# Three chained blocks on one core: values for the block means turned, x turned in chunks, row-wise maxima, nine weight places, shorter routing, first item in parts

## The chip, the cores and the metric

One core of one Trainium2 chip runs the whole program in one launch. The metric is device microseconds (us) of that core from start to end; lower is better. The engines are TensorE (PE, with its weight loads as PEld), VectorE (DVE), ScalarE (ACT), GpSimd (POOL) and SyncE (SP), which here only issues transfers. All of them run their own instruction streams and meet at semaphores.

## The reference

Three blocks follow each other; each takes what the one before gives. The sizes are B=4, H=8, S=768, D=64 for attention, N=3072 tokens of 512 for the two expert blocks, 8 experts of 512x1024 and 1024x512, and 32 slots.

```python
# attention: a local band and 24 block summaries
k_sum = k.reshape(B, H, nb, 32, D).max(axis=3)
v_sum = v.reshape(B, H, nb, 32, D).mean(axis=3)
scores_l = scale * q @ k^T, kept where |i - j| < 16
scores_s = scale * q @ k_sum^T + log(32)
a = softmax over both together;  x = a @ [v, v_sum]
# soft mixture: slots are softmax-weighted means of tokens, per column
logits = x @ phi
d = softmax over tokens (axis 0);  slot_input = d.T @ x
slot_out[e] = relu(slot_input[e] @ w1[e]) @ w2[e]
x = softmax over slots (axis 1) @ slot_out
# switch: one expert per token, gated by its probability
logits = normalised x @ normalised expert_emb.T / tau
out[mask_e] = gate * (relu(x[mask_e] @ w1b[e]) @ w2b[e])
```

## The kernel before

**Attention.** Per batch the 8 heads go as 4 pairs, each pair as 3 steps (NSTEP = 12 a batch, 48 in all). A step scores 4 tiles of 128 rows against 96 near keys and 24 block keys (120 columns). On PE a step is: scores of step s+2 (a mask product and 8 small ones, L539, L547), the transposes of the probabilities of s+1 (L556), the products with the values of s (L569). DVE takes the row maximum (L949), scales it (L953) and, when the products are there, divides (L970 to L977). ACT does the exponentials (L806) and the copy of the transposed probabilities (L814). So each step passes PE, DVE, ACT, PE, ACT, PE, and scores run two steps ahead. The block maxima of keys are taken by DVE (L944) and spread by POOL into gaps between the key windows (L455, "gaps_filled").

**Block sums of v.** They come from a second copy of v laid out by block (v_by_block, 96 partitions of 16384 B a batch). DVE halves one part for the first batch; POOL halves the rest (L439) and spreads the sums (L449). Then SP copies them into rows 48 to 72 of every value window by DMA (load_sums, L341); for this the windows are loaded in two pieces of 48 partitions (L327, L328).

**The order of transfers.** All of them are issued by SP in one program order. A wait on one holds up all behind it. Keys and queries of pair p of batch b (L320) wait until the scores of the same pair one batch earlier are done, values until its products are done. The weights are 16 units of 2 MB in a ring of 8 places (load_unit, L262); units 0 to 3 are issued inside attention, 4 when the scores of the last pair but one are over, 5 to 7 once the logits are done, 8 to 15 as soft_up and the second product free places.

**Soft mixture.** PE turns x (96 transposes, L598), waits for all copies, and multiplies with phi (L605). The maximum of each slot over all tokens is a maximum per row, turned, reduced and sent back (L612 to L618) before the exponentials (L834). They are turned (L621), copied, multiplied with x (L630). Then per pair of experts: soft_up (L659), relu, transposes, second product (L700). The exponentials of the combine weights, their transposes and a copy (L843) stand before the first soft_up.

**Switch routing.** A Gram matrix and logits of slots (L716), then products with the combine weights (L723) give the squared norm and the logits of each token; the norms, the softmax and the choice of expert are made in one row of DVE instructions (L1081 to L1100), then counted (L727), then the list of experts used is made (L1109 to L1126, experts_ready), and only then SP loads w1b of that expert (L389) and, behind it, w2b.

**Items.** An item is 256 tokens of one expert. In these inputs all tokens go to one expert, so n_used is 1 and there are 12 items. The inner matrices are folded, g = slot_out @ w1b (L744), and split into a high and a low part for three products in the fast 32-bit form (L774, 24 for each tile of 128 tokens); hidden is L760. w2b is split the same way by ACT (L910) and DVE (L1202). Items are walked by each_item: a loop over 8 groups of 12 with a branch for each group and each item. Each finished tile is gated by ACT (L876) and scattered by POOL (L516).

## Time and profile before

| | |
|---|---|
| median of 3 runs | 481.75 us (481.75 to 485.83) |
| the profiled execution | 482.98 us, its span 481.2 us |
| granted clock, mean over the span | 0.865 |
| PE busy | 347.4 us, 72% |
| DVE, ACT, POOL busy | 191.3, 147.2, 73.9 us |
| HBM read | 68.91 MB |
| chain that ended last | PE 52%, DMA 25%, DVE 9% |

The rows further down are of four kinds. A stage table has, for each stretch of the span, the busy time of each engine with its number of instructions, the granted clock of TensorE (1 is 2.4 GHz, 0.5 is 1.2 GHz), the busy share of the DMA engines and what they moved. The chain of waits is the one line of work, followed back from the end, that set the end; a DMA row in it is time in which everything waited for that transfer. A timeline lists the instructions of one engine with their start and length, and in brackets how long the engine was idle before and who ended it.

### The profile page before, as it was taken

The page shows a single profiled execution, that of the slowest core. Times are in us where ns is not written, and L with a number is a line of the kernel's source. Part 1 is how long each engine was busy: PE and PEld are TensorE (multiplying, and loading weights), DVE is VectorE, ACT ScalarE, POOL GpSimd, SP SyncE. Part 2 cuts the span into 40 slices and gives each one's busy share as a digit, 9 for nine tenths or more (in the row PEclk, how much of TensorE's full clock was granted, in tenths as well). Part 3 has the DMA queues.
Part 4 walks back from the last instruction along what each step waited for, and adds up shares of the span by engine and source line. Part 5 has one row for each costly group of instructions (what it writes and reads, how often), then busy time and mean ns, then how long its engine had stood idle before and what let it go on. Part 6 is the DMA issues. An engine that isn't in the chain of part 4 may idle for free.

```text
span 481.2 us, 8929 instructions
## 1 busy us (share of the span) xinstructions
PE 347.4 (72%) x3119; PEld 243.7 (51%) x3120; DVE 191.3 (40%) x435; ACT 147.2 (31%) x329; POOL 73.9 (15%) x103
## 2 busy tenths in 40 slices
PE   0516737399689697958871850438999999999991
PEld 0314525266456465733320330117888888888880
DVE  1614435268777477443110138263222222222221
ACT  1203325066367375341200011052222222222221
POOL 3302600811710030000000000000111111111110
PEclk9967768599799799977977895567999999999997
DMA  8999999979999822076799800900111111111110
GB/s 228 254 250 290 386 227 216 224 199 240 229 243 315 196 94 84 1 268 256 293 377 406 320 1 0 330 22 1 44 44 44 44 44 44 44 44 47 49 49 29
DMA packets 23174, 77.90 MB, mean 162 GB/s; under 512 B 2376, under 2 KB 3528, under 8 KB 22768
## 3 DMA queue, kind: packets, MB, share of 16 engines
q1 hardware_dynamic: 21232, 71.31, 50.5%
q0 software_dynamic: 1920, 6.29, 3.4%
q8 instruction: 14, 0.23, 0.2%
q14 instruction: 8, 0.07, 0.0%
HBM read 68.91 MB, written 6.29 MB: 156 GB/s over the span
## 4 chain that ended last, share of the span: by engine, by line
PE 52%; DMA 25%; DVE 9%; issue 4%; ACT 3%; SPq 3%; POOL 1%; DVEq 0%; ACTq 0%; POOLq 0%
PE ps L774 28%; DMA ring<-ring 9%; DMA ring<-in_qk 8%; DMA ring<-in_moe_w 6%; DMA ring<-vsum 3%; PE ps L569 3%; PE ps L659 3%; PE ps L760 2%; PE ps L556 2%; PE ps L700 2%; PE ps L547 2%; DVE small L949 2%; PE ps L598 2%; ACT work L806 2%; PE ps L630 2%
## 5 line engine op out<-in xcount | busy, mean ns | idle before, releaser
L806 ACT ACTIVATE work<-ps,small 128x120 f32<-128x120 f32 x192 | 53.4, 361 | 106.2 <-DVE small L953 106.1
L774 PE MATMUL ps<-high_w2b,hid_high 128*128 x192 | 76.0, 396 | 4.7 <-DVE hid_low L1176 4.7
L774 PE MATMUL ps<-low_w2b,hid_high 128*128 x192 | 75.7, 394 | 0.0
L774 PE MATMUL ps<-high_w2b,hid_low 128*128 x192 | 75.4, 393 | 0.0
L1176 DVE SCALAR_TENSOR_TENSOR hid_low<-ps,hid_high 128x1024 fp32r<-128x1024 f32 x26 | 31.8, 1225 | 61.8 <-ACT hid_high L894 61.8
L569 PE MATMUL ps<-ring,work 120*64 120x65 f32 x768 | 37.4, 247 | 25.6 <-DMA ring<-ring 15.3
L556 PE MATMUL ps<-ident,work 128*120 128x128 f32 x192 | 35.4, 313 | 19.7 <-ACT work L806 19.2
L516 POOL DMA_INDIRECT out_x<-work,small x24 | 23.5, 979 | 166.9 <-DVE small L1169 59.6
L876 ACT ACTIVATE work<-ps,small 128x512 f32<-128x512 f32 x24 | 16.5, 688 | 104.3 <-PE ps L774 104.3
L569 PEld LDWEIGHTS ps<-ring,work 120*64 120x64 f32 x768 | 30.3, 155 | 35.1 <-issue 27.0
L774 PEld LDWEIGHTS ps<-high_w2b,hid_high 128*128 128x128 f32 x192 | 36.6, 191 | 12.2 <-issue 5.0
L774 PEld LDWEIGHTS ps<-high_w2b,hid_low 128*128 128x128 f32 x192 | 36.6, 190 | 7.9
L774 PEld LDWEIGHTS ps<-low_w2b,hid_high 128*128 128x128 f32 x192 | 36.7, 191 | 7.2
L556 PEld LDWEIGHTS ps<-ident,work 128*120 128x120 f32 x192 | 22.5, 152 | 30.7 <-ACT work L806 26.6
L949 DVE TENSOR_REDUCE small<-ps 128x4 f32<-128x480 f32 x48 | 31.4, 655 | 13.8 <-PE ps L547 13.2
L539 PE MATMUL ps<-work,ident_bf 128*128 128x240 bf16 x96 | 21.0, 307 | 21.8 <-POOL ring L455 21.8
L547 PE MATMUL ps<-ring 64*64 64x120 f32 x768 | 36.5, 314 | 0.0
L439 POOL TENSOR_TENSOR ring<-ring 96x512 f32<-96x512 f32 (+5 forms) x16 | 29.5, 1842 | 34.9 <-DMA ring<-in_v_by_block 34.2
L659 PE MATMUL ps<-ring,small 128*32 128x512 f32 x128 | 20.7, 812 | 15.0 <-DMA ring<-in_moe_w 14.4
L547 PEld LDWEIGHTS ps<-ring 64*64 64x64 f32 x768 | 23.7, 155 | 12.1 <-issue 12.1
L814 ACT ACTIVATE work<-ps 120x512 f32<-120x512 f32 x48 | 29.5, 614 | 0.3 <-PE ps L556 0.3
L1165 DVE CAST g_stage<-g_parts 128x1024 fp32r x14 | 9.7, 694 | 47.8 <-PE ps L760 46.0
(193 smaller groups left out, 339.8 us busy)
## 6 DMA issues: line engine op xcount, KB each, us to landing
ring<-in_moe_w SPq DMA_DIRECT2D x17, 2048.0 KB, 14.9
ring<-in_qk SPq DMA_DIRECT2D x16, 928.0 KB, 16.7
ring<-in_v SPq DMA_DIRECT2D x32, 292.5 KB
ring<-in_v_by_block SPq DMA_DIRECT2D x4, 1536.0 KB, 14.1
whole_w2b<-in_moe_w SPq DMA_DIRECT2D x1, 2048.0 KB, 12.6
ring<-ring SPq DMA_DIRECT2D x12, 146.2 KB
ring<-vsum SPq DMA_DIRECT2D x4, 146.2 KB
out_x<-work,small POOLq DMA_INDIRECT x24, 2.7
```

The costliest lines, as they stand in the source:

```text
L439: link(pool.tensor_tensor(left, left, right, ALU.add))
L516: pool.indirect_dma_start(out, bass.IndirectOffsetOnAxis(id_buf[u], 0), o_sb[u], None, bounds_check=NTOK - 1, oob_is_err=False).then_inc(r ...
L539: pe.matmul(sc[u][:, h, 0:2 * KC], ident_bf[:, :], mask[:, 2 * g:2 * g + 2, :].rearrange("p i c -> p (i c)"), start=True, stop=False, skip ...
L547: last = pe.matmul(sc[u][par * QT:(par + 1) * QT, h, ii * KC:(ii + 1) * KC], qT[pair][rows, (2 * i + par) * QT:(2 * i + par + 1) * QT], kT ...
L556: last = pe.transpose(pt[s % 2][0:KC, j, :], probs[s % 2][:, j, :], ident[:, :])
L569: last = pe.matmul(av_of(u, h, ii)[par * QT:(par + 1) * QT, :], probsT[u][0:KC, 2 * h + ii, par * QT:(par + 1) * QT], v_win[pair][0:KC, t, ...
L659: last = pe.matmul(ps[j * SLOTS:(j + 1) * SLOTS, pr % 2, :], siT[:, c, :], as_w1(4 * pr + j // 2)[:, c, (j % 2) * BANK:(j % 2 + 1) * BANK] ...
L774: last = pe.matmul(ps[:, 4 + u, :], hidden_part[:, u, m * P:(m + 1) * P], matrix[:, bass.ds(e * UNIT + m * DM, DM)], start=m == 0 and i == ...
L806: last = act.activation(probs[u][:, j, :], sc[u][:, j // 2, (j % 2) * KC:(j % 2 + 1) * KC], ACT.Exp, bias=negmax[u][:, j:j + 1], scale=flo ...
L814: act.activation(probsT[s % 2][0:KC, :, :], pt[s % 2][0:KC, :, :], ACT.Copy).then_inc(pT_ready, 1)
L949: dve.tensor_reduce(topscore[s % 2].rearrange("p (h i) -> p h i", h=2), sc[s % 2][:, :, 0:2 * KC].rearrange("p h (i c) -> p h i c", i=2), ...
L1176: dve.scalar_tensor_tensor(hid_low[:, u, :].rearrange("p (m t) -> p m t", t=P), hidden_of(u), 0.0, hid_high[:, u, :].rearrange("p (m t) -> ...
```

## The change

- **v turned.** The copy of v by block is replaced by one with the head dimension on 128 partitions (vt, 3072 B a row). DVE halves the first pair, POOL the other 15 (halve). PE turns the 24 sums of a pair (sums_by_block), DVE copies them (copy_block_sums), POOL writes them into the windows (fill_sums). No sums go by DMA.
- **Windows.** Value windows are loaded as one piece of 128 partitions. The stride of the key windows is 120 in place of 88, so a row of queries and keys is 8832 B in place of 7424 B; the block keys stand behind each window.
- **Masks and maxima.** The mask product is 4 quarter-array products in place of 2 full ones. The unscaled maximum lies in PSUM. The 1e-9 comes from a 121st row, so one DVE instruction goes from each step.
- **Issue.** ACT issues the first two vt loads, emb, tau and phi. Units 0 and 1 go after pair 1 and pair 2 of batch 1, 2 and 3 behind the last attention load; there is a ninth place for unit 8, in the space of x.
- **x in chunks.** The transposes of one chunk of 128 columns are followed by the logits of an earlier chunk; the first two stand inside the last two attention steps.
- **Row-wise maxima.** Exponentials use the maximum of their own row and read PSUM; a factor per row sets them to the common maximum later. The combine weights are made behind the first second product.
- **Routing.** The expert is chosen from logits without norms; the first expert is known from one short reduction, and its w1b is loaded in 4 parts, w2b in 4 more. Norms and gates come after the split of w2b.
- **First item.** Its first tile does all high-high products, then low-high, then high-low. keep_at_work adds products whose result nobody reads (5, 4, 2 and 1 of them).
- **Loops.** each_rank and each_item branch once for the case of one expert.

```diff
-            def load_blocks(b):
-                if b > 1:
-                    sp.wait_ge(vsum_pool, b)
-                sp.dma_start(v_blk, v_by_block[b].rearrange("p (j d) -> p j d", j=BLOCK)).then_inc(vblk_loaded, 16)
...
-                rows = v[b, pair].rearrange("p (t d) -> p t d", t=NT)
-                sp.dma_start(v_win[pair][0:FIRST, :, :], rows[0:FIRST]).then_inc(v_loaded[pair], 16)
-                sp.dma_start(v_win[pair][FIRST + NB:KC, :, :], rows[FIRST:WK]).then_inc(v_loaded[pair], 16)
...
-                sp.dma_start(v_win[pair][FIRST:FIRST + NB, :, :], source).then_inc(v_loaded[pair], 16)
+                sp.dma_start(v_win[pair], v[b, pair].rearrange("p (t d) -> p t d", t=NT))\
+                    .then_inc(v_loaded[pair], 16)
...
+                if n >= 2:
+                    if n > 2:
+                        sp.wait_ge(vb_ready, n - 2)
+                    else:
+                        sp.wait_ge(first_vb, 1)
+                    sp.dma_start(vT[n % 2], vt[b, pair]).then_inc(vT_loaded[n % 2], 16)
...
+            def halve(n):
+                pool.wait_ge(vT_loaded[n % 2], n // 2 * 16 + 16)
+                if n >= 2:
+                    pool.wait_ge(vsum_done, n - 1)
+                t = vT[n % 2]
+                for w in (16 * NB, 8 * NB, 4 * NB, 2 * NB):
+                    link(pool.tensor_tensor(t[:, 0:w], t[:, 0:w], t[:, w:2 * w], ALU.add))
+                pool.tensor_tensor(vb[n % 2][:, 0:NB], t[:, 0:NB], t[:, NB:2 * NB], ALU.add).then_inc(vb_ready, 1)
...
-        topscore = [small[:, 1032 + 4 * u:1036 + 4 * u] for u in range(2)]
+        topscore = [flat[:, (2 * u + 1) * BANK - 4:(2 * u + 1) * BANK] for u in range(2)]
...
+            def keep_at_work(bank, times):
+                for _ in range(times):
+                    pe.matmul(ps[:, bank, :], ident[:, :], comb[:, 0:BANK // SLOTS, :].rearrange("p q s -> p (q s)"),
+                              start=True, stop=True)
...
-            with eng.Fori(0, E) as c:
-                with eng.If(c * NPT < n_items):
-                    with eng.Fori(0, NPT) as j:
-                        with eng.If(c * NPT + j < n_items):
-                            body(c * NPT + j)
+            with eng.Fori(1 if head else 0, NPT) as j:
+                body(j)
+            with eng.If(n_items > NPT):
...
+                elif kidx == 7:
+                    sp.wait_ge(logits_part, DC)
+                elif kidx == RING:
+                    sp.wait_ge(si_done, 1)
+                else:
+                    p = kidx - RING - 1
+                    if p % 4 < 2:
+                        sp.wait_ge(h_done, p // 4 + 1)
+                    else:
+                        sp.wait_ge(so_done, p // 4 + 1)
...
-            act.activation(E_sb, L_sb, ACT.Exp, bias=nmax, accum_out=zpart).then_inc(e_ready, 1)
+            act.activation(E_sb, flat[:, 4 * BANK:4 * BANK + S], ACT.Exp, bias=nmax, accum_out=zpart).then_inc(e_ready, 1)
...
+                for i, (hidden_part, matrix) in enumerate(((high, high_m), (low, high_m), (high, low_m))):
```

The queue of SP before, in batch 1 from behind pair 1 to behind pair 2 ("in_v" are the two pieces of the value window, the ring<-ring row is the copy of the sums):

```order
L315 DMA ring<-in_v_by_block 96x4096 [waits vsum_pool]
L320 DMA ring<-in_qk 128x1856 [waits scores_done]
L327 DMA ring<-in_v 48x1560 [waits av_done]
L328 DMA ring<-in_v 48x1560
L341 DMA ring<-ring 24x1560 [waits vsum_spread,av_done] x3
```

and the start of batch 1 now (in_vt is the turned v; its two places are in the ring and in comb):

```order
L341 DMA ring<-in_qk 128x2208 [waits scores_done]
L351 DMA ring<-in_vt 128x768 [waits vb_ready]
L357 DMA ring<-in_v 128x1560 [waits av_done]
L341 DMA ring<-in_qk 128x2208 [waits scores_done]
L351 DMA comb<-in_vt 128x768 [waits vb_ready]
L357 DMA ring<-in_v 128x1560 [waits av_done]
L277 DMA ring<-in_moe_w 128x4x1024
```

A pair has three transfers of 128 partitions in place of one of 128, two of 48 and one of 24, with one of 96 for each batch; and a vt load waits for POOL's halving two pairs earlier.

PE at the end of attention before (L569 are products with the values, L598 transposes of x, L605 logits):

```order
L556 MATMUL ps<-ident,work 120x128 x4
L569 MATMUL ps<-ring,work 64x65 x16
L598 MATMUL ps<-ident,x_or_g 128x128 x96
L605 MATMUL ps<-ring,phi_sb 32x512 x4
L605 MATMUL ps<-ring,phi_sb 32x256 x4
```

and now (L611 are the products with the values, L624 the transposes, L632 the logits):

```order
L581 MATMUL ps<-ident,work 120x128 x4
L624 MATMUL ps<-ident,x_or_g 128x128 x6
L611 MATMUL ps<-ring,work 64x65 x8
L624 MATMUL ps<-ident,x_or_g 128x128 x6
L611 MATMUL ps<-ring,work 64x65 x8
L624 MATMUL ps<-ident,x_or_g 128x128 x36
L632 MATMUL ps<-work,phi_sb 32x512 x4
L632 MATMUL ps<-work,phi_sb 32x256 x4
L624 MATMUL ps<-ident,x_or_g 128x128 x24
```

Twelve transposes moved ahead of the last products with values, and the other 84 are mixed with the logits.

DVE from the logits of the tokens to the first expert now (before, 35 DVE instructions stand from the same point, L1081, to experts_ready at L1126):

```order
L1248 TENSOR_REDUCE small<-ps 128x24 [waits y_done]
L1249 TENSOR_TENSOR small<-ps,small 128x192 [waits dve_seq]
L1256 TENSOR_REDUCE small<-ps 1x8 [waits count_done,codes_ready]
L1257 SCALAR_TENSOR_TENSOR work<-small 1x8 [waits dve_seq]
L1258 TENSOR_REDUCE small<-work 1x1 [waits dve_seq]
L1259 TENSOR_SCALAR en_home<-small 1x1 [waits dve_seq]
```

Six instructions now stand between them; the norms and gates have moved behind the split of w2b.

## Rows read from the trace of the kernel before

**Rows 1.** Stage table: stretch, busy us (instructions) by engine, clock, DMA share, GB/s.

```profile
34.00:186.00 152.00, 112.19 (x1758) 78.15 (x1760) 89.68 (x243) 73.01 (x227) 41.53 (x53) 0.83 0.90 236
186.00:206.00 20.00, 16.82 (x172) 12.99 (x166) 11.34 (x22) 7.33 (x10) 0.00 (x0) 1.00 0.00 1
206.00:225.00 19.00, 12.68 (x88) 6.35 (x91) 7.98 (x16) 6.24 (x9) 0.00 (x0) 0.82 0.91 331
225.00:281.00 56.00, 40.22 (x296) 13.51 (x295) 6.58 (x12) 4.32 (x7) 0.00 (x0) 0.82 0.80 301
281.00:301.00 20.00, 4.48 (x54) 3.50 (x54) 13.86 (x48) 3.75 (x5) 0.41 (x2) 0.72 0.00 1
301.00:338.00 37.00, 21.49 (x76) 13.76 (x77) 14.09 (x22) 8.84 (x10) 1.09 (x1) 0.64 0.32 115
```

**Rows 2.** Chain of waits in attention: start, length, what.

```profile
21.98 15.04 DMA ring<-vsum
39.01 27.39 DMA ring<-in_qk
73.41 18.73 DMA ring<-ring
```

**Rows 3.** Stage table, single stretches while attention loads or weights are in flight.

```profile
13.00:14.00 1.00, 0.00 (x0) 0.00 (x0) 0.65 (x1) 0.00 (x0) 0.00 (x0) 1.00 1.03 198
16.00:17.00 1.00, 1.00 (x17) 0.70 (x16) 1.00 (x1) 0.00 (x0) 0.96 (x1) 1.00 1.02 423
28.00:29.00 1.00, 0.00 (x0) 0.00 (x0) 0.00 (x0) 0.00 (x0) 0.00 (x0) 0.50 0.99 402
45.00:60.00 15.00, 9.28 (x134) 6.28 (x135) 5.85 (x13) 4.92 (x16) 11.46 (x8) 0.77 1.05 392
```

**Rows 4.** Timeline of PE, first products with values.

```profile
34.04 1.13 PE L569 MATMUL ps<-ring,work 120*64 120x65 f32 x16 [10.29 <-DMA ring<-vsum]
```

**Rows 5.** Timeline of ACT: exponentials of steps, two stretches without a transfer wait.

```profile
99.63 1.11 ACT L806 ACTIVATE work<-ps,small 128x120 f32<-128x120 f32 x4 [2.03 <-DVE small L953]
...
115.66 1.11 ACT L806 ACTIVATE work<-ps,small 128x120 f32<-128x120 f32 x4 [1.04 <-DVE small L953]
...
176.76 1.11 ACT L806 ACTIVATE work<-ps,small 128x120 f32<-128x120 f32 x4 [0.77 <-DVE small L953]
...
183.12 1.11 ACT L806 ACTIVATE work<-ps,small 128x120 f32<-128x120 f32 x4 [0.48 <-DVE small L953]
```

**Rows 6.** Timelines of POOL and DVE at the same moment.

```profile
119.51 4.51 POOL L439 TENSOR_TENSOR ring<-ring 96x2048 f32<-96x2048 f32 x1 [2.53 <-DMA ring<-in_v_by_block]
...
119.73 4.32 DVE L953 TENSOR_SCALAR small<-small 128x4 f32<-128x4 f32 x1
```

**Rows 7.** Groups by line and form: busy, mean ns, idle before.

```profile
L439 POOL TENSOR_TENSOR ring<-ring 96x512 f32<-96x512 f32 x4 | 5.3, 1334 | 0.2
L449 POOL COPY ring<-vsum 96x1560 f32<-96x1560 f32 x3 | 4.4, 1480 | 9.0 <-DMA ring<-ring 8.9
L953 DVE TENSOR_SCALAR small<-small 128x4 f32<-128x4 f32 x48 | 16.6, 346 | 1.7
```

**Rows 8.** Timeline of PE: transposes of x.

```profile
191.42 8.08 PE L598 MATMUL ps<-ident,x_or_g 128*128 128x128 f32 x72 [0.89 <-DVE ring L1018]
```

**Rows 9.** Chain of waits, last two pairs of experts.

```profile
246.30 18.96 DMA ring<-in_moe_w
265.39 5.56 PE ps L659 x32
```

**Rows 10.** Timelines of SP, PE and DVE from the load of w1b on.

```profile
300.73 0.39 SPq L389 DMA_DIRECT2D ring<-in_moe_w  x1
308.62 6.15 PE L744 MATMUL ps<-ring,soT 128*64 128x512 f32 x16 [5.12 <-DMA ring<-in_moe_w]
319.21 4.62 DVE L1202 TENSOR_TENSOR low_w2b<-whole_w2b,high_w2b 128x1024 fp32r<-128x1024 f32 x4
```

**Rows 11.** Chain of waits, one item of 12.

```profile
346.85 10.91 PE ps L774 x48
```

More of the change, by code:

```diff
@@ L110, in attention_soft_moe_switch_moe @@
         x_sb = x_or_g[:, :].rearrange("p (b t d) -> p b t d", b=B, t=TT)
+        vb = [small[:, 1416 + SLAB * u:1416 + SLAB * (u + 1)] for u in range(2)]
         L_sb = work[:, 0:768]
@@ L704, in _ @@
                 last.then_inc(so_done, 1)
+                if pr == 0:
+                    comb_T()
+                for n in range(NCT):
+                    if ct_turn(n) == pr:
+                        if n == 1:
+                            embeddings_T()
+                        combine_T(n)
+                if 1 <= pr < E // 2 - 1:
+                    soft_up(pr + 1)
             pe.wait_ge(so_ready, 1)
@@ L724, in _ @@
             last.then_inc(y_done, 1)
[L726 to L727 removed]
+            pe.wait_ge(topped, 1)
+            pe.matmul(ps[:, 6, 0:NI], ones_bf[:, :], onehot.rearrange("p q e -> p (q e)"),
                       start=True, stop=True).then_inc(count_done, 1)
[L730 to L733 removed]
@@ new lines, in _, with list_T @@
+            for t in range(TT):
+                last = pe.matmul(flat[:, 4 * BANK + t * P:4 * BANK + (t + 1) * P], combT[:, t * P:(t + 1) * P],
+                                 gram_bd.rearrange("p b s -> p (b s)"), start=True, stop=True)
+            last.then_inc(gram_done, 1)
+            keep_at_work(3, 4)
+            def list_T():
+                pe.wait_ge(items_ready, 1)
+                for kind in range(3):
+                    last = pe.matmul(ps[0:1, 6, kind * P:(kind + 1) * P], item[:, kind:kind + 1],
+                                     ident[:, :], start=True, stop=True)
+                last.then_inc(list_done, 1)
@@ new lines, in _ @@
+            with dve.If(n_used < FEW + 1):
+                low_of_w2b(0, 0)
+                stage(1, (g_low_ready, n_used * 2))
+                low_part(0, 0)
+                for c in range(1, 4):
+                    low_of_w2b(0, c)
+                low_part(0, 1)
+                with dve.If(n_used > 1):
+                    for r in range(1, FEW):
+                        with dve.If(n_used > r):
+                            for c in range(4):
+                                low_of_w2b(r, c)
@@ L1208, in _ @@
+            with dve.If(n_used < FEW + 1):
                 each_item(dve, one_item(low_part))
             with dve.If(n_used > FEW):
-                stage(1, (hid_done, 1))
-                for u in range(2):
-                    second_half(0, u)
                 each_item(dve, one_item(second_half))
```

887 lines of the change are left out of this document (498 added, 389 removed).

## Prediction

> **What bounds the kernel now.** I read the stage table first, to cut the span where the limits change [rows 1]. Attention runs to 186, with the DMA engines 90% busy at only 236 GB/s while PE is busy 112 of 152 us. Turning x and the logits take until 206, soft routing until 225, the expert weights until 281 (80% DMA share at 301 GB/s), the choice of expert until the load of w1b at 300.7 [rows 10], the first item until 338. Then the items fill PE, 48 products in 10.91 us [rows 11] and the hidden ones between them, 143 us in all; the change leaves these products alone.
>
> Next the chain of waits in attention [rows 2]: one wait of 15.0 us for sums going by DMA, one of 27.4 us for keys, and one of 18.7 us for copies of sums, the longest of three (one for each later batch). So transfers set the end there, not arithmetic. Where no transfer is waited for, steps start 2.29 us apart (7 steps in 16.03) or 2.12 us (3 steps in 6.36) [rows 5].
>
> Why only 236 GB/s: the single stretches [rows 3] alternate. Keys and queries, 128 partitions high, come at 423 and 402 GB/s and the weights at 392, but in between, when by issue order the value pieces of 48 partitions are moving, it is 198. The Trainium skill, "SBUF — State Buffer", section "Door 1: The DMA port swizzle", says that partitions 0 to 63 lie on 8 of the 16 ports and 64 to 127 on the others, so that a piece of 48 gets about half the rate; the trace agrees (198 against 423). The same page puts HBM at about 358 GB/s for a core, and here the measurement, 392 over 15 us, decides; by the page attention would end some 6 us later than below.
>
> **The change part by part.** Against the span of 481.2 us.
>
> *Transfers of attention.* A pair loads keys and queries 8832 B x 128 = 1.13 MB, values 6240 B x 128 = 0.80 MB, vt 3072 B x 128 = 0.39 MB: 2.32 MB, in all 37.2 MB, against 33.5 MB now (0.95 + 0.60 + 0.15 a pair and 1.57 a batch). More bytes, but all in transfers of 128 partitions. At the 402 of rows 3 a pair takes 5.8 us, less than its three steps. With units 0 and 1 (2.1 MB each) it is 41.4 MB, 103 us, over by about 106, while the last pair is wanted near 119. So the waits of rows 2 go, and the loop of steps is what bounds next.
>
> *The loop of steps.* Per pair DVE loses three instructions on the sums and gains one copy of sums; PE gains one turning product; the quarter-array mask products cost between nothing and what they now cost. These go together; I take 2.25 us a step, near the 2.29 which has the block maximum in it. Bounds 2.12 and 2.45.
>
> *Start.* PE stood ready for the first products at 34.04 - 10.29 = 23.75 [rows 4]. Ahead of and with the first keys 2.5 MB had to land at about 200 GB/s, 12.6 us; now 1.9 MB at 402, 4.8 us. That gives 16, and the first sums add some 2 us: 18. Bounds 16 and 21. The last products end at 18 + 47 x 2.25 + 0.7 = 124.5. Gain 61.5.
>
> *POOL.* It is moved into every pair: 744 elements of additions at 2.6 ns (1334 ns for 512 [rows 7]) are 1.9 us, the copy of sums 1.5 us, the gaps 0.4: about 4 us of 6.75, so it does not bound. Behind each halving SP holds a vt load and all loads after it, but two pairs (13 us) lie between them.
>
> *x and logits.* 84 transposes instead of 96 remain (8.08/72 = 0.112 us each [rows 8], -1.3 us), and PE is idle 3.2 of these 20 us [rows 1], waiting for DVE at the start, for banks and for all copies before the logits; 2.7 of it goes. Gain 4, bounds 2 and 5.
>
> *Soft routing.* 19 us [rows 1]. A copy, a table load and half of another copy leave the path; at ACT's mean there (6.24/9 = 0.7, the table load about twice that) this is 2.5. DVE's round trip for the common maximum goes from it (two instructions at 7.98/16 = 0.5), and six transposes of combine weights trade places with six of logits. This sums to 3.5; PE stands idle for less time before the products with x and is at the low clock for less of them (mean 0.82 now), so 4.5. Bounds 2 and 6.
>
> *Expert weights.* Unit 8 starts at the end of the products with x. From the first soft_up (T) it is 3.8 us to its end, then units 9 to 15, 7 x 2.1 MB at 402 = 36.6 us, about 2 us to land: T + 42.4. Before, the chain waited 18.96 us for unit 13 and ran 15.6 us on PE behind it to 281 [rows 9]. Now unit 13 lands at T + 32, its soft_up takes 5.56 us cold or 3.6 warm, turning and copies 2.3, then five unread products of 0.85 (twice that at the low clock), ending T + 44; then 3.6 us: T + 48 against T + 56. Gain 8. The unread products cost about 2 us here, since the last weights land earlier; without this cover, up to 6. Bounds 4 and 11.
>
> *Choice of expert and first item.* DVE's 35 instructions between logits and list become 6 before the first expert is known. From 281 to the load of w1b at 300.7 it was 19.7 us, of which DVE 13.86 in 48 instructions, 0.29 each [rows 1]. Now some 9 of them are on the path (2.6), with 3.8 of products and 1.1 for SP: 7.5. The parts land until 7.8 us after the issue, so of the 6.15 us of products behind it [rows 10] only the last quarter is left, under 1.5 us. Then hidden, its high part, and four low parts of w2b (4.62 us [rows 10]) bound the first tile, done 20 us after the issue; the second needs its low part at 21 and ends at 27.5. **A wait is added:** behind that low part DVE has about 18 small instructions for ids, norms and gates (near 7 us), and everything of item 1 is queued behind them, so item 1 starts at about 32, with PE idle for 4 to 5 us. Before it was 37.3. Both together gain 12.2 + 5.3 = 17.5; I take 15.5 for a low clock after that idle time. Bounds 9 and 20.
>
> *End.* The seven branches of empty item groups behind the last item go; no row prices a branch, so I bound it by nothing and 4 us (the last product ends about 10 us before the span does) and take 2.
>
> Sum: 61.5 + 4 + 4.5 + 8 + 15.5 + 2 = 95.5. The span goes to 385.7; with 1.8 us around it the profiled execution would be 387.5. It lies 1.2 us above the median of 481.75, so 386 for the median.
>
> **The rivals.**
>
> *The value rows are slow in themselves.* 6240 B is no multiple of 256, and 198 GB/s was never seen on another length with 128 partitions. Then a pair takes 2.8 + 4.0 + 1.0 = 7.8 us, with two units 135 us, attention ends at 149 and the total is 411. For it: the new windows have the same row length; against it: the halves explain the number. 0.10.
>
> *POOL holds DVE.* A scaling of 128x4 maxima took 4.32 us beside a POOL addition of 4.51 [rows 6]; its mean is 346 ns [rows 7]. With POOL busy in 60% of each step at instructions of up to 1.5 us, a hold of 0.3 us on average at each of 48 steps, on the loop's path, makes 15 us: 401. The change puts the maxima into PSUM. The Trainium skill, "SBUF — State Buffer", section "Who interferes with whom", says that a VectorE instruction with at most one SBUF input outside the two-port modes does not contend with GpSimd; by that rule this rival falls, but no run here shows it for this operand. 0.11.
>
> *Slower than before: the low clock through the items.* The stretch of the first item is at 0.64 [rows 1], and I expect a new idle time before item 1. If TensorE stayed at 1.2 GHz, each item would take another 10.9 us, 131 in all: 517. It decides when over 96/131, 73% of the items, run so. Against it: the 48 products go at 0.227 us each [rows 11] without a gap, and nothing in the loop of items changed. 0.02.
>
> *The gains do not chain* (loads late in a place I have not seen, the unread products worse): 0.05, spread over 395 to 440.
>
> **How the numbers follow.** The forecast has 0.72 and gives 386. Its own range from the bounds, not all at one end, is 370 to 402. The low end stays; the high end takes in the first two rivals: 370 to 411. A measurement of this kernel can tell about 1% from no change, so same is 477 to 487. Faster 0.96, same 0.01, slower 0.03.
>
> **What would show it.** In the profile after: no wait for sums or keys in the chain of attention, step starts 2.1 to 2.4 us apart throughout, the last products near 125; the short stretches near 400 GB/s whenever loads run; DVE's scaling well under its mean of 346 ns beside POOL; the last weights landing before the fifth unread product ends; PE idle 4 to 5 us before item 1. It would be wrong if value loads stay near 200 GB/s, or if steps take over 2.5 us with no transfer in the chain.

## The result, and the profile after

The kernel after takes 386.12 us (median of 4 runs, 383.76 to 389.18), the kernel before 482.88 (481.75 to 485.83): ratio 0.799, 95% interval 0.792 to 0.807. Forecast were 386.0 and a span of 385.7; the profiled execution spans 385.7. The sum came out closer than its terms did. Some executions of any kernel run in a slower state, and ratios here and below compare the fast ones alone. The kernel before was run again beside each series of experiments, with medians from 482.9 to 485.7 us, and the kernel after was not. So a microsecond or two between kernels of different series is not to be read as their edits'; where it matters, the lines of the profiles are compared instead.

The stage table of after stands beside [rows 1]; its columns are the same, cut where the same stages now end.

```profile
0.00:16.00 16.00, 6.80 (x74) 4.38 (x75) 6.37 (x15) 4.92 (x15) 9.76 (x29) 1.00 0.84 319
16.00:123.00 107.00, 95.95 (x1895) 72.09 (x1894) 79.14 (x214) 73.70 (x229) 67.20 (x126) 0.98 1.02 412
123.00:139.00 16.00, 15.19 (x148) 10.71 (x147) 9.53 (x13) 5.68 (x7) 0.00 (x0) 1.00 0.49 183
139.00:151.00 12.00, 9.30 (x81) 4.45 (x81) 3.57 (x12) 3.04 (x7) 0.00 (x0) 1.00 0.66 210
151.00:201.20 50.20, 42.81 (x316) 14.91 (x308) 13.26 (x27) 7.74 (x12) 0.00 (x0) 0.93 0.87 327
201.20:209.00 7.80, 5.54 (x65) 5.20 (x65) 3.45 (x16) 0.60 (x1) 0.42 (x2) 0.80 0.00 0
209.00:245.70 36.70, 28.07 (x104) 15.87 (x103) 23.17 (x55) 11.43 (x15) 1.13 (x1) 0.90 0.32 116
245.70:385.70 140.00, 132.35 (x616) 110.67 (x616) 37.17 (x56) 37.12 (x45) 22.37 (x24) 0.98 0.12 45
```

Second line: attention is now 107 us, the transfers run at 412 GB/s without a break, and PE is busy 96 of them. The low mean of 236 GB/s is gone, and so are the long waits of [rows 2]. The chain of waits of after (start, length, what) has two transfers left in attention, one at the start and one of vt:

```profile
1.38 9.30 DMA comb<-in_vt
...
16.02 1.07 PE ps L611 x16
...
35.44 12.61 DMA ring<-in_vt
48.17 1.01 POOL ring L484
```

First value products at 16.02, against a forecast of 18 (34.04 before, [rows 4]); the last start at 122.29, 47 steps later, 2.26 us each. The second transfer is where the pace broke once: TensorE stood still 1.6 us near 50 and then ran at the low clock until about 56 (granted clock 0.56 from 53 to 56). Behind the hitch, from 63.63 to 122.22, 27 steps go at 2.17 us each.

From the second pair of soft experts on, the same chain reads:

```profile
169.20 6.55 PE ps L764 x32
...
191.64 0.67 PE ps L754 x4
...
193.07 4.56 PE ps L704 x10
197.63 3.62 PE ps L764 x32
...
208.86 0.36 SPq L401
...
210.88 6.81 DMA ring<-in_moe_w
...
217.74 0.81 PE ps L812 x6
218.55 1.01 PE ps L827 x4
219.56 3.75 issue
223.31 3.44 PE ps L704 x4
226.75 0.96 PE ps L857 x8
...
239.01 0.37 DVE small L1388
...
243.98 1.23 DVE hid_low L1331
...
245.68 4.57 PE ps L871 x12
```

Between the first soft_up at 150.73 and the choice of expert the chain has no transfer at all: TensorE and VectorE set the pace there, and the second product at 169.20 runs at the low clock, 6.55 us instead of the 3.64 of the others. `193.07 4.56 PE ps L704 x10` are the five unread products, whole on the chain; the prediction counted them and put 2 us on them. `219.56 3.75 issue` answers to nothing in the prediction. It is time in which TensorE waited for nothing that the profile shows, and behind it unread products at half speed (3.44 us instead of 1.98) push the first hidden tile from about 222 to 226. The last lines are the wait that the prediction named: item 1 starts at 245.68, after 4.19 us of idle TensorE (timeline of PE):

```profile
245.68 0.49 PE L871 MATMUL ps<-high_w2b,hid_high 128*128 x1 [4.19 <-DVE hid_low L1331]
```

VectorE's small instructions end at 240.71. The 5 us behind them are ScalarE's way into the loop of items (registers and branches, 1.6 us), its copies, and the high and low part of the tile.

### The profile page after: what moved, and what is told of

Its sections match the earlier page's. It is cut to its first block, busy times and chain, and to the rows that moved or that the text cites. A ratio compares the mean times of both kernels' runs of the same rounds, so it can differ in the third digit from the quotient of the medians.

```text
span 385.7 us, 9018 instructions
## 1 busy us (share of the span) xinstructions
PE 336.0 (87%) x3282; PEld 238.3 (62%) x3283; DVE 175.6 (46%) x405; ACT 144.2 (37%) x329; POOL 100.9 (26%) x181
## 4 chain that ended last, share of the span: by engine, by line
PE 65%; DVE 12%; DMA 7%; ACT 5%; issue 5%; POOL 3%; ACTq 1%; SPq 1%; DVEq 0%; POOLq 0%
PE ps L871 32%; PE ps L611 4%; PE ps L581 4%; PE ps L725 4%; PE ps L764 4%; DMA ring<-in_vt 3%; ACT work L929 3%; PE ps L857 3%; PE ps L624 3%; DMA comb<-in_vt 2%; DVE ps L1090 2%; PE ps L704 2%; DMA ring<-in_moe_w 2%; PE ps L572 2%; PE ps L632 1%
## 5 line engine op out<-in xcount | busy, mean ns | idle before, releaser
L871 PE MATMUL ps<-high_w2b,hid_high 128*128 (+1 forms) x184 | 72.4, 394 | 4.2 <-DVE hid_low L1331 4.2
L871 PE MATMUL ps<-low_w2b,hid_high 128*128 (+1 forms) x184 | 72.4, 393 | 0.0
L871 PE MATMUL ps<-high_w2b,hid_low 128*128 (+1 forms) x184 | 72.3, 393 | 0.0
L611 PE MATMUL ps<-ring,work 121*64 121x65 f32 x768 | 33.8, 232 | 0.0
L611 PEld LDWEIGHTS ps<-ring,work 121*64 121x64 f32 x768 | 27.1, 141 | 8.9 <-issue 4.5
L1090 DVE TENSOR_REDUCE ps<-ps 128x4 f32<-128x480 f32 x48 | 31.8, 662 | 1.6 <-PE ps L572 1.1
L572 PE MATMUL ps<-ring 64*64 64x120 f32 x768 | 30.4, 278 | 0.0
L466 POOL COPY ring<-vsum 24x1560 f32<-24x1560 f32 x16 | 23.8, 1486 | 25.0 <-DVE vsum L1107 22.2
L1024 ACT ACTIVATE hid_high<-ps 128x1024 fp32r<-128x1024 f32 x26 | 26.6, 1023 | 7.3 <-PE ps L857 5.0
L1126 DVE TENSOR_TENSOR x_or_g<-ps,small 128x256 f32 (+1 forms) x48 | 20.4, 425 | 5.6 <-DVE small L1121 0.2
## 6 DMA issues: line engine op xcount, KB each, us to landing
ring<-in_v SPq DMA_DIRECT2D x16, 780.0 KB, 10.3
```

The source lines that it names most:

```text
L466: pool.tensor_copy(v_win[pair][WK:KC, :, :], sums).then_inc(sums_filled, 1)
L572: last = pe.matmul(sc[u][par * QT:(par + 1) * QT, h, ii * KC:(ii + 1) * KC], qT[pair][rows, (2 * i + par) * QT:(2 * i + par + 1) * QT], kT ...
L611: last = pe.matmul(av_of(u, h, ii)[par * QT:(par + 1) * QT, :], probsT[u][0:KC + 1, 2 * h + ii, par * QT:(par + 1) * QT], v_win[pair][0:KC ...
L871: last = pe.matmul(ps[:, 4 + u, :], hidden_part[:, u, m * P:(m + 1) * P], matrix[:, bass.ds(e * UNIT + m * DM, DM)], start=m == 0 and i == ...
L1024: act.activation(hid_high[:, u, :].rearrange("p (m t) -> p m t", t=P), hidden_of(u), ACT.Relu)\
L1090: dve.tensor_reduce(topscore[s % 2].rearrange("p (h i) -> p h i", h=2), sc[s % 2][:, :, 0:2 * KC].rearrange("p h (i c) -> p h i c", i=2), ...
```

## Experiments

**1 and 2. Height of a transfer, or length of its rows?** Both split each value window into two transfers, by partitions or by columns (the waits on them, left out here, count two instead of one).

```diff
-                sp.dma_start(v_win[pair], v[b, pair].rearrange("p (t d) -> p t d", t=NT))
+                rows = v[b, pair].rearrange("p (t d) -> p t d", t=NT)
+                for half in (slice(0, P // 2), slice(P // 2, P)):        # experiment 1
+                    sp.dma_start(v_win[pair][half, :, :], rows[half]) ...
+                for half in (slice(0, NT // 2), slice(NT // 2, NT)):     # experiment 2
+                    sp.dma_start(v_win[pair][:, half, :], rows[:, half]) ...
```

> The kernel after, with each value window loaded as two transfers of 64 partitions (0 to 63, then 64 to 127), same rows of 6240 B, same bytes. Theory (the number of partitions that a transfer covers sets its rate, as with 198 GB/s against 402 before): each half moves at about 200 GB/s, so the values of a pair take 4.0 us instead of 2.0, a pair takes some 7.7 us of DMA against 6.65 us of steps, and the transfers become the bound of attention: the last value products end near 145 instead of 122.9, and the run takes 403 to 412 us. Rival (row length or something else in the value windows made them slow before, not the height): no change beyond 1 us, since the kernel after moves the same rows at full rate.

> The kernel after, with each value window loaded as two transfers of all 128 partitions, each with half of the columns (3120 B a row). It has as many transfers, issues and semaphore counts as the run with two halves of the partitions. Theory (height of a transfer): full rate, attention ends within 1 us of 122.9, run 385 to 388. Rival (more transfers or shorter rows cost the time): attention slower by several us, as in the other run.

Measured: halves of the partitions 439.8 us (one run, last value products at 179.75), column parts 383.6 (last at 122.51). Single microseconds from the stage table of the run with halves:

```profile
60.00:61.00 1.00, 1.00 (x22) 0.88 (x23) 0.51 (x2) 0.78 (x3) 0.00 (x0) 0.50 0.95 391
...
62.00:63.00 1.00, 1.00 (x30) 0.80 (x32) 0.36 (x2) 0.57 (x3) 0.00 (x0) 1.00 1.19 160
63.00:64.00 1.00, 0.86 (x24) 0.64 (x16) 0.00 (x0) 1.00 (x4) 0.00 (x0) 1.00 0.88 135
...
65.00:66.00 1.00, 0.00 (x0) 0.00 (x0) 0.00 (x0) 0.00 (x0) 0.00 (x0) 1.00 1.07 191
66.00:67.00 1.00, 0.00 (x0) 0.00 (x0) 0.25 (x1) 0.00 (x0) 0.00 (x0) 1.00 0.98 202
```

and of the run with column parts:

```profile
16.00:123.00 107.00, 94.64 (x1887) 71.19 (x1884) 78.89 (x213) 73.83 (x232) 67.19 (x126) 0.98 1.03 409
```

The same bytes in as many transfers: 409 GB/s if each covers 128 partitions, and 268 GB/s over 18 to 180 us with halves in between, with the DMA engines busy throughout (1.03). Of the 22 single microseconds from 60 to 82, nine lie between 135 and 202 GB/s. Height decides, and row length (6240 or 3120 B) does not; each kernel ran once, but they lie 56 us apart. By the Trainium skill, "SBUF — State Buffer", section "Door 1: The DMA port swizzle", a half reaches 8 of 16 ports; the 191 and 202 agree. But the run came out 28 us above even the theory's range. Measured, a step took (179.75 - 18.0) / 47 = 3.44 us (first value products at 18.0), 10.3 a pair. The 7.7 of the expectation had left out the two units, 0.7 a pair; that is a slip of mine. The rest is the rate: if the half-height bytes (at most 12.8 MB) moved at 198 GB/s and the others at 402, the 43.4 MB of 18 to 180 us would take at most some 141 us, an estimate from these rows, and they took 162. With 160 and 135 GB/s there are stretches well under half the rate. Why the mean falls under what the two rates give is not settled.

**3. Does GpSimd hold VectorE?**

```diff
-        topscore = [flat[:, (2 * u + 1) * BANK - 4:(2 * u + 1) * BANK] for u in range(2)]
+        topscore = [small[:, 1032 + 4 * u:1036 + 4 * u] for u in range(2)]
```

> The kernel after, with the row maxima written to SBUF again instead of to PSUM, so that the scaling of 128x4 maxima reads and writes SBUF while GpSimd is at work in each pair. Rival of the prediction (GpSimd holds VectorE): the scaling, 162 ns now, has a mean of 400 ns or more with single ones over 1 us, each hold delays the exps, attention takes 5 to 15 us more, and the run 391 to 401. Other reading (the 4.32 us before was a single case that needs something else, such as a two-port mode): mean stays under 200 ns and the run is within 1 us of 386.

Measured: 384.3 us (one run). Groups by form on VectorE in attention, with the maxima in SBUF, then in the kernel after (count, busy us, mean ns):

```profile
L1094 DVE TENSOR_SCALAR small<-small 128x4 f32<-128x4 f32 x44 | 13.1, 297 | 1.5
```

```profile
L1094 DVE TENSOR_SCALAR small<-ps 128x4 f32<-128x4 f32 x45 | 7.3, 162 | 1.5
```

Both readings are half right. The place of the operand matters: 297 against 162 ns beside the same GpSimd work, with single ones of up to 735 ns (in SBUF). But 6 us of VectorE's time are not 6 us of the end: the last value products start at 123.11 instead of 122.22. The 0.9 understates it a little, because this execution kept the high clock behind its own hitch near 50 (granted 1.00 from 50 to 56, in after 0.72). Over the last 27 steps, with no hitch in either, it takes 60.1 us instead of 58.6, so the whole is some 2 us. The rival at 401 would not have come even without the move into PSUM. On the mechanism, the section "Who interferes with whom" of the Trainium skill's "SBUF — State Buffer" lists `tensor_scalar` among the operations that can enter a two-port mode and then contend; the longer mean fits that, though no run here shows which mode was taken. The prediction had weighed only its rule on the number of inputs.

**4. The one hitch of attention.**

```diff
-    EARLY_BEHIND = ((1, 1), (2, 1), (3, 3), (3, 3))
+    EARLY_BEHIND = ((2, 1), (3, 1), (3, 3), (3, 3))
```

> The kernel after, with the first two soft-expert units loaded behind pairs (2,1) and (3,1) instead of (1,1) and (2,1). Theory: at about 410 GB/s the transfers of a pair take 5.7 us against 6.65 of steps, so the backlog of the start shrinks by 1 us a pair; a unit of 5 us put in as early as (1,1) meets a backlog that is still there, which makes the vt load at 35.4 land 12.6 us after its issue and leaves TensorE waiting 1.6 us at 49.5 and then at the low clock for 4 us. Later units remove that one wait: the last value products end 2 to 3 us earlier (about 120.4), run about 384. Rival (the backlog comes back with each unit, wherever it is): the hitch moves to another place and the end of attention stays within 0.5 us of 122.9.

Measured: 379.7 us (one run); the vt transfer is gone from the chain, the last value products start at 119.31, 2.9 us earlier. The theory holds, and the hitch did not move elsewhere. The other 3.5 us of the difference to 386.1 I do not put down to this edit: its profile has no gap behind the products with w1b (experiments 9 and 12), and from the end of the last second product to item 1 it takes 39.2 us instead of the 44.5 of after's profile.

**5. The unread products before the last weights.**

```diff
-                if pr == E // 2 - 1:
-                    keep_at_work(5, 5)
```

> The kernel after without the five unread products that stand ahead of the last second product of the soft experts. In the profile of the kernel after they run from 193.07 to 197.6, while the transfers of the last weights end near 193.9. Theory (the last weights bound there, the unread products only stand in front): the last second product starts at 194 to 194.5 instead of 197.6, still at the high clock since the turning before it ended at 192.3, and everything behind it comes 3 to 3.5 us earlier; run 382.5 to 383. Rival (the unread products buy the clock): after the thin stretch from 191 to 194 the last second product runs at the low clock, 6.5 us instead of 3.6 as at 169.2, and so do the choice of expert and the waits behind it; gain 0 to 1 us or a loss of up to 2.

Measured: 388.87 us (4 runs, 386.27 to 389.91; ratio to before 0.804, 0.800 to 0.809). Timeline of PE (start, length, line, idle before and what ended it):

```profile
192.06 0.65 PE L754 MATMUL ps<-ident,work 128*128 128x128 f32 x4 [0.81 <-ACT work L971]
196.17 5.23 PE L762 MATMUL ps<-ring,work 128*32 128x512 f32 x32 [3.46 <-DMA ring<-in_moe_w]
```

The rival holds in the main. The weights landed at 196.17, not 193.9, which is 45.0 us behind the first soft_up of this run (151.14). In after, whose first soft_up is at 150.73, that makes 195.8, so the five products (to 197.6) cost 1.9 us, close to the 2 us of the prediction. Without them the idle 3.46 us bring the last second product to the low clock for part of its length, 5.23 us instead of 3.64, and the gain is gone. Both profiled executions have a gap behind the products with w1b (3.20 and 3.75 us) and they differ by 0.6 us (388.14 and 387.55). The medians of four lie 2.7 us apart, but the runs overlap, so I do not read that as the edit's.

**6. The wait before item 1.** VectorE's ids go ahead of the copy of the list; norms and gates between the first stage copy and the low parts, with ScalarE's exponential ahead of its first high part.

```diff
                 low_of_w2b(0, 0)
                 stage(1, (g_low_ready, n_used * 2))
+                norms()
                 low_part(0, 0)
-                for c in range(1, 4):
+                low_of_w2b(0, 1)
+                gate_values()
+                for c in range(2, 4):
                     low_of_w2b(0, c)
```

> The kernel after with VectorE's small instructions for token numbers, norms and gates moved out from behind the low parts of the first item: the numbers to where VectorE waits for the list (near 216), norms and gates to between the stage copy (223.6) and the low part of the first hidden tile (228.8). My step of the prediction (the added wait: everything of item 1 is queued behind them, TensorE idle 4 to 5 us in front of item 1, measured 4.19) says that this idle time goes whole: item 1 starts right behind the last product of item 0 and at the high clock, run 4.5 to 5.5 us shorter, 381. Rival (the idle time only changes its owner: o_sb, ids or ScalarE's gated copy and high part release item 1 too late anyway): idle time of 2 us or more is left before item 1, gain under 2.5 us.

Measured: 382.42 us (4 runs, 381.89 to 383.38; ratio to before 0.792, 0.789 to 0.795). In the timeline of PE the products of item 0 and item 1 now follow each other at 0.23 us, with no idle time (last product of item 0, first of item 1):

```profile
242.33 0.39 PE L871 MATMUL ps<-high_w2b,hid_low 128*128 128x512 f32 x1
242.56 0.39 PE L871 MATMUL ps<-high_w2b,hid_high 128*128 x1
```

The step of the prediction is shown: the moved instructions held item 1. The gain is 3.7 us, less than the 4.5 to 5.5 expected: on ScalarE the exponential now stands ahead of the high part of the first tile, and TensorE waits 1.32 us there.

**7. What the parts are worth.**

```diff
-            for c in range(DC):
-                sp.dma_start(as_w1(0)[:, c, :], ...).then_inc(w1b_part[c], 16)
+            sp.dma_start(as_w1(0), w1b[bass.ds(e0, 1)] ...).then_inc(w1b_part[0], 16)
```

(w2b in the same way.)

> The kernel after with the first expert's two matrices loaded as one transfer each instead of four, and all waits on the whole. It leaves the earlier issue and the order of the first item as they are. By the sum of the prediction the parts are worth 4.6 us on w1b (6.15 us of products behind the last arrival against under 1.5), and on w2b what the first tile waits for its high and low parts. Theory: from the issue of w1b to item 1 it takes 3 to 6 us more, run 389 to 392. Rival (the products are short at the high clock, 4.3 us for all sixteen, and the clock is lost in the wait in either case, so the parts save little): 0 to 2 us more.

Measured: 388.7 us (one run). From the end of the last second product (202.6) to item 1 (246.50) it takes 43.9 us, in maxima_in_sbuf, which has no gap behind the products with w1b, 39.2 (201.95 to 241.16). So the parts are worth 4.7 us, inside the 3 to 6. The timeline of PE shows how: nothing can start before the whole of w1b has landed, and all sixteen products stand behind it.

```profile
218.93 4.13 PE L823 MATMUL ps<-ring,soT 128*64 128x512 f32 x12 [3.10 <-DMA ring<-in_moe_w]
222.99 1.13 PE L808 MATMUL ps<-ident,small 128*1 128x128 f32 x6
...
227.35 1.21 PE L853 MATMUL ps<-cT,g_parts 128*128 x8
```

**8. Why GpSimd does the halving.** The four additions and the last one of each pair on VectorE, after the second step of a pair:

```diff
-                if n + 1 < B * NPAIR:
-                    halve(n + 1)                 # GpSimd
+                    if s % NG == 1:
+                        ahead(halve, b, s // NG + 2, NPAIR, last_batch)   # VectorE
```

> The kernel after with the halving of the turned values (four additions and a last one per pair) on VectorE instead of GpSimd; the copies of sums and gaps stay on GpSimd. GpSimd takes 2.7 us a pair for them, in parallel. VectorE was busy 84.9 of 101 us in attention, so 16 us are free there. Theory (VectorE lies on the path of the loop of steps): additions of 384, 192, 96, 48 and 24 elements take about 0.45, 0.3, 0.2, 0.15 and 0.15 us, 1.25 us a pair and 19 for 15 pairs, most of it on the path: attention 8 to 17 us longer, run 394 to 403. Rival (steps are bound by the round trip between engines, the halving falls in VectorE's idle time): attention within 3 us, run under 389.

Measured: 407.3 us (one run), last value products at 140.75, 18.5 us later. Groups by form on VectorE:

```profile
L1099 DVE TENSOR_TENSOR ring<-ring 128x384 f32<-128x384 f32 x7 | 3.8, 548 | 0.0
...
L1099 DVE TENSOR_TENSOR ring<-ring 128x192 f32<-128x192 f32 x7 | 2.5, 358 | 0.2
...
L1101 DVE TENSOR_TENSOR small<-ring 128x24 f32<-128x24 f32 x7 | 1.3, 184 | 0.2
```

With 258 and 208 ns for the two between, 0.55 + 0.36 + 0.26 + 0.21 + 0.18 = 1.56 us a pair, 23 for 15 pairs, of which 18.5 reach the end. GpSimd takes longer for the same (2.5 us for four of them), and in after's chain its additions stand only at the start and up to the hitch near 50. The chain of waits of this run has the additions on it (19% of the stretch from 60 to 120). So VectorE lies on the path of the loop although in after it is busy only 79 of 107 us; the share of busy time does not tell this. The cost is a little above the range expected (8 to 17 us, run 394 to 403), and this profile has a gap of 3.26 us behind w1b besides.

**9. The gap.** TensorE reads the number of experts and branches before it waits for w1b:

```diff
-            expert_in(0)
             n_used = load_experts(pe)
             with pe.If(n_used > 1):
+                expert_in(0)
                 for r in range(1, E):
                     with pe.If(n_used > r):
                         expert_in(r)
+            with pe.If(n_used < 2):
+                expert_in(0)
```

> The kernel after with one thing moved: TensorE reads the number of experts in use and branches ahead of the first expert's products (while it still waits for w1b) instead of behind them; where only one expert is in use, as here, the code of the seven other experts is skipped there. In some profiled executions TensorE stood still 3.06 to 3.75 us with nothing released to it right behind these products (after at 219.6, no_five_unread_products, norms_and_ids_early), in others not at all (maxima_in_sbuf), and the executions of the kernel after spread from 383.8 to 389.2. Theory (the branch over that code has to wait for instructions, which an execution has or has not at hand): the idle time moves under the wait for w1b, no idle time of over 1 us is left between the last product with w1b and the first hidden tile, median 383 to 384 and a spread under 2.5 us. Rival (the gap belongs to something behind the branch, such as the register loads ahead of the hidden products): it stays where it is, median 385.5 to 387 and the same spread.

Measured: 384.85 us (6 runs, 383.9 to 386.43; ratio to before 0.800, 0.795 to 0.806). Its timeline of PE, beside the lines from 218.55 on of after's chain above:

```profile
216.99 2.79 PE L827 MATMUL ps<-ring,soT 128*64 128x512 f32 x12 [0.94 <-issue]
...
220.46 1.08 PE L827 MATMUL ps<-ring,soT 128*64 128x512 f32 x4
221.47 1.98 PE L704 MATMUL ps<-comb,ident 128*128 128x512 f32 x4
223.76 1.21 PE L859 MATMUL ps<-cT,g_parts 128*128 x8 [0.31 <-DVE g_parts L1311]
```

The gap left its place with the branch: it is 0.94 us now and stands ahead of the products. The spread is 2.5 us instead of 5.4. The median lies 1.3 below after's, a little more than forecast and not to be told from it by these runs. Of the nine profiled executions so far with the branch in its old place, four have the gap (3.06 to 3.75 us: after, experiments 5, 6 and 8) and five have none. The transfers of instructions (queue 8) do not decide it: in after one falls into the gap, at 220, but in maxima_in_sbuf and v_in_two_column_parts one moves near 221 and there is no gap. The Trainium skill, "Runtime: NRT & Kernel Launch", section "Instruction fetch mechanics", says that a taken branch to a target outside the instructions at hand forces a fetch before the engine goes on; no run here shows such a fetch by itself. So experiment 12 took the code away instead of moving the branch.

**12. No code to branch over.** TensorE's first products of experts 1 to 7 are left out (they never run with this input):

```diff
             n_used = load_experts(pe)
-            with pe.If(n_used > 1):
-                for r in range(1, E):
-                    with pe.If(n_used > r):
-                        expert_in(r)
```

> The kernel after without TensorE's code for the first products of the seven other experts and its branches (left out: these products; with one expert in use, as here, they never run). The read of the number of experts stays where it was. Theory (the gap of 3.06 to 3.75 us is a wait for instructions behind a branch over this code, some 120 instructions and more): with nothing to jump over, the profile has no idle time above 1 us between the last product with w1b and the first hidden tile, the median is 383 to 384 and the spread of the runs under 2 us, below skip_before_w1b (384.85, where the branch is only moved). Rival (the gap belongs to the register read or to what comes behind): idle time of 3 us there again, median 385.5 to 387.

Measured: 383.98 us (6 runs, 382.89 to 386.07). Timeline of PE:

```profile
219.59 1.08 PE L827 MATMUL ps<-ring,soT 128*64 128x512 f32 x4
220.59 1.98 PE L704 MATMUL ps<-comb,ident 128*128 128x512 f32 x4
222.90 1.21 PE L853 MATMUL ps<-cT,g_parts 128*128 x8 [0.32 <-DVE g_parts L1305]
```

The register read is still there, the gap is not, and the median is as forecast. With only one profile, and five profiles without a gap though they have the code, this fits the theory and doesn't prove it. The cause of the gap stays open: that it moves with the branch is seen in experiments 9 and 11, that it is a wait for instructions is argued. The spread of 3.2 us, more than the 2 expected, says that something else varies as well.

**10 and 11. The steps joined.**

> The kernel after with four edits together: units 0 and 1 behind pairs (2,1) and (3,1); the skip ahead of the products with w1b; VectorE's norms ahead of the copy of the list (the token numbers and gates stay behind the low parts); three unread products instead of five ahead of the last second product, so that they end about when its weights land at T + 45.4. From the single runs: 2.9 us from the units (attention ended at 120.0 instead of 122.9), 1.4 from the unread products with the high clock kept, 3 to 3.5 of the 4.19 us of idle time before item 1, and 0 to 3.7 from the skip. If they add up: 376 to 377.5. Rival (moved work lands on a new wait: the norms delay the list or the low parts of the expert by up to 1 us, the earlier end of attention only makes the weights bound, whose loads depend on the ring and not on attention): 379 to 381.

> The kernel joined_steps, and in attention the turning product of the next pair's sums behind the first value products of a pair instead of ahead of them, with GpSimd filling the sums of pair 0 before it halves pair 1. In the kernel after the chain at the start runs over vt of pair 1 (landed at 10.7), its halving on GpSimd (2.7 us) and the filling of sums (1.5) to the first value products at 16.02, though the sums of pair 0 were ready at 11.0. Theory: first value products at about 14.2, and 1.5 to 2 us of it reach the end: 1 to 2 us below joined_steps. Rival (the steps behind it are bound by keys of the next pairs or by the exps, so the start is given back within the first pairs; or the later turning product delays sums in every pair): within 0.5 us of joined_steps, or slower.

Experiment 10 joins the edits of 4 and 9, `keep_at_work(5, 3)` for `(5, 5)`, and the norms; its new part, and that of 11 (which also puts `sums_by_block` of the next pair behind the value products of a pair):

```diff
+            dve.wait_ge(x_norms, 1)                  # 10, up to lexp_in: moved to here
+            newton(nrm, n2, newton_t)
             ...
             dve.wait_ge(list_done, 1)
-            halve(1)                                 # 11
             fill_sums(0)
+            halve(1)
```

Measured: joined_steps 378.13 us (6 runs, 375.12 to 381.13; ratio 0.786, 0.779 to 0.793), joined_steps_and_start 377.14 (375.08 to 378.95; ratio 0.784, 0.778 to 0.789). Both ran in one series. In joined_steps idle time before item 1 is down from 4.19 to 1.04 us, attention ends 2.8 us earlier, the three unread products end 1.44 us before the weights land, and the last second product keeps its 3.64 us. Forecast were 376 to 377.5 and by the rival 379 to 381; the median lies between them, 8.0 us of about 9. The changed start brought the first value products to 15.24 only, not 14.2, and the last ones 0.7 us earlier, less than the 1.5 to 2 expected of the end. The median is 1.0 lower, but the runs overlap, so theory and rival are not told apart. Its profile also shows that the gap is not cured, only moved ahead of the products with w1b:

```profile
205.07 4.08 PE L704 MATMUL ps<-comb,ident 128*128 128x512 f32 x8
212.55 0.87 PE L827 MATMUL ps<-ring,soT 128*64 128x512 f32 x2 [3.41 <-issue]
```

From the end of the last second product to item 1 it takes 41.1 us here and 38.7 in joined_steps, whose profile has no gap, so there the gap costs some 2.5 us; behind the products it cost 5.3 (44.5 against 39.2). In joined_steps the last second product reads:

```profile
192.98 3.64 PE L764 MATMUL ps<-ring,work 128*32 128x512 f32 x32 [1.44 <-DMA ring<-in_moe_w]
```

The last version beats both kernels: all its 6 runs lie below the lowest of after (383.76) and of skip_before_w1b, which ran in the same series (383.9). joined_steps still spreads over 6.0 us, so its mean gain is sure and the size of it is not.

## Where the prediction was right, and where its terms were off

- **Attention**, forecast gain 61.5, measured 63 (last products from about 186 to 122.9). The transfers ceased to bound, as argued; experiment 1 undoes this alone and gives the time back. The start was 2 us better than forecast, the pace 2.26 instead of 2.25, with the hitch in it. One sentence there doesn't follow from its own sum: at 358 GB/s the 41.4 MB would be over by about 119, when the last pair is wanted, and not end attention 6 us later. Measured are 412 GB/s.
- **x and logits**, forecast 4, measured 3.5 (122.9 to 139.2; before 186 to 206). **Soft routing**, forecast 4.5, measured 7.3: the way to the products with x got 4.6 us shorter, not 3.5; the 48 products took 5.36 us at the high clock instead of 7.27, where I had allowed 1 us; and 0.7 came behind them.
- **Expert weights**, forecast 8 (T + 48, T being the first soft_up, now at 150.73), measured 5.6 (T + 50.5). Two steps failed. The unread products, whose end sets this stage, were to be over at T + 44 and were over at T + 46.9. The prediction let the last soft_up start when its weights land, at T + 32; it started at 187.26, T + 36.5, behind TensorE's own earlier work. VectorE makes the combine weights and the rows of the experts between 159 and 166, so that TensorE is busy only 2.78 of the 6 us from 163 to 169, and the second product behind it is at the low clock, 2.9 us longer than the others. No term had this. And the last weights were to land at T + 42.4; they landed at T + 45.0 (in experiment 5 and in joined_steps alike; for after I take it over). Unit 9 was asked for at T + 3.7, as forecast, but only 172 and 209 GB/s moved from 155 to 157, and 396 from 157 to 193 instead of 402; the rest of the 2.6 us is not traced. With the landing as forecast the stage would still have ended at T + 50.5; with the path of TensorE as forecast and the landing at T + 45, near T + 48.6. So the first step is what cost the 2.5 us. The unread products cost 1.9 us, forecast 2.
- **Choice of expert and first item**, forecast 15.5, measured 12.6. The step up to the issue of w1b was exact (7.6 us, forecast 7.5), and so was the idle time before item 1 (4.19, forecast 4 to 5). What was missing is the gap of 3.75 us, which some executions have, with the unread products at half speed behind it; where it is absent, from the end of the second products to item 1 took 39.2 us instead of 57.0 before (281 to 338), a gain of 17.8.
- **End**, forecast 2, measured 3.2, of which 2.7 lie behind the last product.

Sum of the measured terms: 63 + 3.5 + 7.3 + 5.6 + 12.6 + 3.2 = 95.2, forecast 95.5 (the stage borders are read to 0.3 us). Errors of 1.5, 2.8 and 1.2 us to one side met 0.5, 2.4 and 2.9 to the other; that the total was exact is luck. Errors of this size with signs at random would leave some 5 us, so the 386 could as well have been 381 or 391.

The rivals: slow value rows fall by experiment 2, a held VectorE falls by experiment 3 in its effect (not in its mechanism), and the low clock through the items did not come (0.98 over the last 140 us).

## What to carry to other kernels

Before trimming bytes, look at how many partitions each transfer covers: this kernel moves more bytes than before, in transfers of 128 partitions, and that alone is worth over 50 us (experiment 1). Which engine gets an operation is decided by whose time is on the path, not by who is faster: the halving is slower on GpSimd and 18 us cheaper there. Products that keep TensorE at work in front of a late transfer did best when they ended 1.4 us before it landed (joined_steps, last second product 3.64 us); without them the clock took back what the idle wait would save (5.23 us), and with five of them they were the wait themselves, for 1.9 us.

## What the runs showed of the hardware

Half-height transfers of values did worse than half the rate for their bytes: 162 us for what 198 and 402 GB/s would move in some 141. TensorE stood still 3.06 to 3.75 us behind a branch over much code in four profiled executions of nine, with nothing released to it; with the branch moved the gap was in the new place (0.94, 3.41 and none), and in the one profile without code to branch over it was absent. VectorE's small scaling takes 162 ns from PSUM and 297 from SBUF while GpSimd works, and that is worth some 2 us over 48 steps. Idle stretches of 3.46 us (before the last second product without unread products) and of 0.94 us after thin work (163 to 169) were followed by the low clock, one of 1.44 us was not.
